# Where ScalarE and VectorE copy the turned attention weights in the first mixed step, and where TensorE turns them in the second

## What is computed

```python
scores = scale * q @ k.T;  scores = where(causal, -1e9, scores)
a = exp(scores - scores.max(-1));  a /= a.sum(-1) + 1e-9
local = a @ v
mem_out = (phi(q) @ M_prev) / (phi(q) . z_prev + 1e-6)
x = g * mem_out + (1 - g) * local            # rows of 512

h = x @ w_in                                  # layer 1, 512 -> 1024
sm = exp(h - h.max(-1));  sm /= sm.sum(-1) + 1e-9
solu = h * sm
ln = (solu - mean) / sqrt(var + 1e-6) * g_ln
x = ln @ w_out                                # 1024 -> 512

out = (sigmoid(x @ w_gate) * (x @ w_val)) @ w_out2   # layer 2
```

## Time and profile before

| What | Value |
|---|---|
| median of three runs | 836.41 us (835.51 to 836.73) |
| the profiled execution's own time | 835.18 us |
| its span | 833.4 us |
| time around the span | 1.8 us |
| TensorE (PE) busy | 814.7 us, 98% |
| VectorE (DVE) busy | 604.4 us, 73% |
| ScalarE (ACT) busy | 465.4 us, 56% |
| GpSimd (POOL) busy | 20.7 us, 2% |

### The profile page before, as it was taken

The page is one execution under the profiler, slowest core; times in us unless marked ns, Lnnn a source line. Parts: engine busy times, 40 slices in busy tenths (PEclk is TensorE's granted clock), DMA queues, the critical chain, the costliest instruction groups (busy, mean ns, idle before and its releaser), DMA issues.

```text
span 833.4 us, 15447 instructions
## 1 busy us (share of the span) xinstructions
PE 814.7 (98%) x5718; PEld 688.1 (83%) x5718; DVE 604.4 (73%) x1460; ACT 465.4 (56%) x965; POOL 20.7 (2%) x35
## 2 busy tenths in 40 slices
PE   7997999999999999999999999999999999999998
PEld 4555777777777778888899999999999999999997
DVE  7988888777777775686656777787677678666654
ACT  7988666666666653463535454564444465444443
POOL 1000000000000000111000000000000000000000
PEclk9999999999999999999999999999999999999999
DMA  7362011111111000100323011122111113111002
GB/s 217 93 194 61 17 52 53 53 52 54 53 50 39 26 17 15 52 1 1 101 77 126 26 51 52 52 61 98 45 52 50 52 42 111 51 52 51 26 1 77
DMA packets 67370, 48.99 MB, mean 59 GB/s; under 512 B 9568, under 2 KB 57952, under 8 KB 67296
## 3 DMA queue, kind: packets, MB, share of 16 engines
q1 hardware_dynamic: 67152, 47.74, 19.2%
q10 hardware_dynamic: 144, 0.26, 0.1%
HBM read 43.27 MB, written 4.72 MB: 58 GB/s over the span
## 4 chain that ended last, share of the span: by engine, by line
PE 89%; DVE 5%; SPq 2%; issue 2%; ACT 1%; DMA 1%; DVEq 0%; ACTq 0%
PE tt_bk L1622 10%; PE tt_bk L1624 10%; PE tt_bk L1623 10%; PE m_bk L1467 9%; PE s_bk L1491 7%; PE o_bk L1491 5%; PE tt_bk L1390 4%; PE s_bk L1674 3%; PE s_bk L1675 3%; PE s_bk L1673 3%; PE o_bk L1398 3%; PE s_bk L1326 3%; PE m_bk L1674 2%; PE m_bk L1675 2%; PE s_bk L1467 2%; PE m_bk L1673 2%
## 5 line engine op out<-in xcount | busy, mean ns | idle before, releaser
L1622 PE MATMUL tt_bk<-xc_hi,wc_hi 128*128 128x384 f32 x476 | 160.0, 336 | 0.0
L1624 PE MATMUL tt_bk<-xc_hi,wc_lo 128*128 128x384 f32 x476 | 160.0, 336 | 0.0
L1623 PE MATMUL tt_bk<-xc_lo,wc_hi 128*128 128x384 f32 x476 | 159.8, 336 | 0.0
L598 ACT ACTIVATE p_nat<-p_nat,negmax 128x512 f32<-128x512 f32 (+2 forms) x144 | 83.0, 578 | 46.6 <-DVE negmax L931 46.6
L1166 DVE TENSOR_TENSOR wc_lo<-wc_raw,wc_hi 128x768 fp32r<-128x768 f32 x72 | 78.3, 1088 | 31.9 <-ACT wc_hi L663 31.9
L1622 PEld LDWEIGHTS tt_bk<-xc_hi,wc_hi 128*128 128x128 f32 x476 | 89.4, 188 | 6.4 <-DVE c_u L1182 0.3
L1623 PEld LDWEIGHTS tt_bk<-xc_lo,wc_hi 128*128 128x128 f32 x476 | 89.4, 188 | 6.1
L1624 PEld LDWEIGHTS tt_bk<-xc_hi,wc_lo 128*128 128x128 f32 x476 | 89.4, 188 | 0.0
L663 ACT CAST wc_hi<-wc_raw 128x768 fp32r<-128x768 f32 x72 | 64.5, 946 | 1.3 <-DVE wc_raw L1160 1.3
L605 ACT COPY pT<-tt_bk 128x512 f32<-128x512 f32 (+1 forms) x87 | 46.0, 554 | 29.2 <-PE tt_bk L1390 27.8
L1390 PE MATMUL tt_bk<-ident,p_nat 128*128 128x128 f32 x400 | 56.0, 277 | 2.6 <-DVE pT L975 1.4
(11 more groups left out here) (219 smaller groups left out, 1773.7 us busy)
## 6 DMA issues: line engine op xcount, KB each, us to landing
wc_raw<-in_moe_w_val SPq DMA_DIRECT2D x36, 256.0 KB, 3.0
wc_raw<-in_moe_w_gate SPq DMA_DIRECT2D x36, 256.0 KB, 3.4
qkT<-in_q SPq DMA_DIRECT2D x15, 288.0 KB, 2.9
v_raw<-in_v SPq DMA_DIRECT2D x16, 256.0 KB, 2.7
qkT<-in_k SPq DMA_DIRECT2D x15, 256.0 KB, 3.2
out<-o_sb SPq DMA_DIRECT2D x15, 256.0 KB, 2.2
w_raw<-in_moe_w_out SPq DMA_DIRECT2D x12, 256.0 KB, 4.7
turned<-in_k SPq DMA_DIRECT2D x32, 72.0 KB, 2.6
```

The lines of the kernel that those rows point to most:

```text
L598: nc.scalar.activation(p_tile(g, tile), p_tile(g, tile), ACT.Exp, bias=negmax[:, n:n + 1], scale=-1.0, accum_out=den[:, n:n + 1]).then_inc ...
L1622: mm(o, hi[:, k, c, :], xc_hi[:, j, c, :], start=start and c == 0, stop=False, skip_group_check=True)
L1623: mm(o, hi[:, k, c, :], xc_lo[:, j, c, :], start=False, stop=False, skip_group_check=True)
L1624: last = mm(o, lo[:, k, c, :], xc_hi[:, j, c, :], start=False, stop=c == 1, skip_group_check=True)
```

## The change

In the first tile's step two copies of turned weights are placed ahead of the rows' maximum and its exponential. VectorE copies fill 3 before `split_w2` and `moe_max` (it did so behind them). Fill 4 is copied by ScalarE instead of VectorE, right behind its copy of fill 2 and ahead of `split_w2` of rows 5 and 6 and of `moe_exp`. TensorE's order in this step is the same as before.

In the second tile's step TensorE does all of `moe_hidden` first and then turns the fills among the groups of `moe_out`, where it had turned fills 0 and 1 and fills 2 and 3 among the hidden products. The orders of ScalarE and VectorE in this step stay as they were. The later steps are unchanged.

```diff
--- before.py
+++ after.py
@@ -71,7 +71,7 @@
     def act_fills(g):
         if g < HP:
             return list(range(NF))
-        return [0, 2, 5, 6] if g == HP else [0, 2, 4, 5, 6]
+        return [0, 2, 4, 5, 6]
 
     def dve_fills(g):
         return [n for n in range(NF) if n not in act_fills(g)]
@@ -807,12 +807,14 @@
                 if t == 0:
                     exp_tile(g, 8)
                 keep_pt(g - 1, 2)
+                if t == 0:
+                    keep_pt(g - 1, 4)
                 if t == 1:
                     feature_relu(g + 1)
                 for f in W2_HI_TILE.get(g, ()):
                     split_w2(f)
                 moe_exp(t)
-                if 4 in act_fills(g - 1):
+                if t:
                     keep_pt(g - 1, 4)
                 keep_pt(g - 1, 5)
                 if t == 0:
@@ -1095,12 +1097,13 @@
                     unit_max(g, 6)
                     split_w2(W2_LO_TILE[g][1])
                 keep_pt(g - 1, 1)
+                if t == 0:
+                    keep_pt(g - 1, 3)
                 if t < 2:
                     split_w2(W2_LO_TILE[g][2 if t == 0 else 0])
                 moe_max(t)
-                keep_pt(g - 1, 3)
-                if t == 0:
-                    keep_pt(g - 1, 4)
+                if t:
+                    keep_pt(g - 1, 3)
                 if t == 1:
                     split_w2(W2_LO_TILE[g][1])
                     split_w2(W2_LO_TILE[g][2])
@@ -1563,28 +1566,45 @@
                     scores(g, 2)
                 if t == 0:
                     scores(g, 3)
-                m = (15, 21) if t == 0 else (18, 24)
-                moe_hidden(t, 12, m[0])
-                turn_p(g - 1, 0)
-                turn_p(g - 1, 1)
-                moe_hidden(t, m[0], m[1])
-                turn_p(g - 1, 2)
-                turn_p(g - 1, 3)
+                if t != 1:
+                    m = (15, 21) if t == 0 else (18, 24)
+                    moe_hidden(t, 12, m[0])
+                    turn_p(g - 1, 0)
+                    turn_p(g - 1, 1)
+                    moe_hidden(t, m[0], m[1])
+                    turn_p(g - 1, 2)
+                    turn_p(g - 1, 3)
                 if t == 0:
                     moe_hidden(t, 21, 24)
-                if t:
+                if t > 1:
                     if g < PAIRS:
                         pe.wait_ge(max_ok, NU * g + NU - 1)
                     else:
                         pe.wait_ge(yt_ok, t - 1)
                     moe_out(t - 1, 0, 6)
-                turn_p(g - 1, 4)
-                turn_p(g - 1, 5)
-                if t:
+                if t != 1:
+                    turn_p(g - 1, 4)
+                    turn_p(g - 1, 5)
+                if t > 1:
                     moe_out(t - 1, 6, 12)
-                turn_p(g - 1, 6)
-                if t:
+                if t != 1:
+                    turn_p(g - 1, 6)
+                if t > 1:
                     moe_out(t - 1, 12, 24)
+                if t == 1:
+                    moe_hidden(t, 12, 24)
+                    turn_p(g - 1, 0)
+                    turn_p(g - 1, 1)
+                    pe.wait_ge(max_ok, NU * g + NU - 1)
+                    moe_out(0, 0, 6)
+                    turn_p(g - 1, 2)
+                    turn_p(g - 1, 3)
+                    moe_out(0, 6, 12)
+                    turn_p(g - 1, 4)
+                    turn_p(g - 1, 5)
+                    moe_out(0, 12, 18)
+                    turn_p(g - 1, 6)
+                    moe_out(0, 18, 24)
                 if t and g < PAIRS:
                     scores(g, 3)
```

## The result

| | Runs | Median | Lowest and highest |
|---|---|---|---|
| before | 22 | 836.14 us | 835.01 to 838.50 |
| after | 22 | 836.96 us | 835.74 to 840.54 |

The ratio of after to before is 1.0016, with an interval of 1.0009 to 1.0024. The time is 0.8 us longer by the medians. By the means it is 1.27 us longer (837.45 against 836.18), since six executions of the changed kernel lie between 838.38 and 840.54 us. They have a mean TensorE clock of 0.990 to 0.992. None of the 82 executions of the kernel before that were timed beside the experiments has that; the longest of these took 837.82 us. (One of the 22 above took 838.50 us, and its clock is not on record.) Without the six the mean is 836.71 us, 0.52 us above before. So there are two things to explain: a shift of about 0.6 us, and now and then 2 to 3 us more.

The account below looks back on a forecast made before the run. TensorE bounds the kernel, but ScalarE and VectorE bound the stretch from 80 to 97 us. Their 0.89 us delay less 0.30 us slack gives +0.59 us: 836.41 + 0.6 = 837.0 us, range 835.6 to 838.0.

Parts of the forecast that it names:

- ScalarE decides the side chain: First tile's step: ScalarE waits for fill 4, so `moe_exp` and the ScalarE/VectorE chain behind it come 0.89 us late.
- (a): Rival: side chain hardly delayed, as fill 4's copy is early or splits shorter; -0.3 us, down to -1.2; chance 0.13.
- (b): Rival: only `moe_max`'s delay of 0.43 us counts, the splits being hidden; +0.1 us, 836.5 us; chance 0.12.
- The chain passes on without loss: From `moe_rows` through `moe_square` and `x_lo` to `y_nat`, no slack eats the 0.89 us delay.
- `weighted` waits for the copies of fills 5 and 6, and comes 0.45 us late: TensorE starts `weighted` at about 81.9 instead of 81.45 us, held by ScalarE's copies behind `moe_exp`.
- A new wait ahead of `moe_out`, 0.5 us: Second tile's step: `moe_out` waits for unit 5's maximum, at 95.66 us, while fills 0 and 1 are turned by 95.2.
- The slack at `y_nat`, 0.30 us: Ahead of TensorE's turn of `y_nat`, 0.30 us of slack takes up part of the side chain's delay.
- The sum of +0.59: Whole kernel: side chain's delay of 0.89 us less 0.30 us of slack at `y_nat`; nothing of the removed waits survives.
- The clock stays at 1.00: Around the longer wait ahead of `weighted`, TensorE's granted clock stays full, as between 77 and 82 us; cost nothing.
- rival (d): Rival: the clock falls after TensorE's longer idle time before `weighted`, costing 1.5 us; +2.1 us, 838.5 us; chance 0.03.

Follow-up runs that it names:

- e3: The changed kernel plus seven matmuls with unread results in TensorE's wait ahead of `weighted`; 837.00 us, ratio 1.0005.
- e4: The changed kernel, but ScalarE copies fill 4 behind the two splits of `w_out` and ahead of `moe_exp`; 836.23 us, ratio 1.0001.
- e2: The kernel before with only TensorE's new order in the second tile's step; 836.00 us, ratio 0.9996.
- a1: The changed kernel, unaltered, traced once more; one run, 839.96 us.
- e7: The kernel before with only the first tile's change, plus seven unread matmuls in TensorE's wait ahead of `weighted`; 836.86 us, ratio 1.0007.
- e8: As e5, and ScalarE also copies `y_nat` ahead of the exponential of `q` in the second tile's step; 835.86 us, ratio 0.9995.
- e1: The kernel before with only the first tile's change of ScalarE and VectorE, TensorE's order as before; 837.06 us, ratio 1.0012.
- e5: On e2, ScalarE makes `x_hi` of the second tile ahead of the last split of `w_out`; 835.94 us, ratio 0.9992.
- e6: On e4, VectorE's copy of fill 3 also goes back behind `moe_max`; fill 4 stays with ScalarE; 836.48 us, ratio 1.0001.
- a2: The changed kernel, unaltered, traced another time; one run, 838.44 us.
- e9: The changed kernel with a third split of `w_out` (row 7) ahead of `moe_exp`, lengthening the wait ahead of `weighted`; 838.49 us, ratio 1.0026.

## Why the prediction was right, and where it was not

The time was 836.96 us where 837.0 was forecast, within 0.2% of before and inside the range. That the two agree to 0.04 us is luck: the forecast started from 836.41 us, the median of three runs, and the median of 22 is 836.14, so the measured difference of the medians is 0.82 us and not 0.6. What bears the forecast out is the shift of 0.61 us in e3, where the clock doesn't fall. The steps fared as follows.

**ScalarE decides the side chain.** Right. The idle stretch ahead of the copy was 0.96 us (forecast 1.0 to 1.1), `moe_exp` was 0.89 us late (forecast 0.89), `moe_max` 0.43 (forecast 0.43), and they do not add up: e4 removes ScalarE's part and leaves VectorE's. Rivals (a) and (b) needed a delay of ScalarE that isn't there, and fall.

**The chain passes on without loss.** Right. The copy of `y_nat` begins 27.98 us behind fill 4 in e3, and began 27.09 behind it (104.40 - 77.31): the whole 0.89 us.

**`weighted` waits for the copies of fills 5 and 6, and comes 0.45 us late.** This step failed. It comes 0.87 us late (5.01 against 81.45 - 77.31 = 4.14), and its releaser is `moe_rows`, not a copy. In the second tile's step TensorE has a wait for `u_ok` ahead of `weighted` (in `step`, for `t` = 1, behind those for the copies), and I read only the waits for the copies. Before, `moe_rows` ended at 81.23 (80.01 + 1.22) and `weighted` started at 81.45, behind it as well. So this start hangs on the side chain, and moves with it: 0.87 of the 0.89 us. The open wait is 2.11 us, not 1.7. For the sum this made no difference, since the wait at `y_nat` swallows either.

**A new wait ahead of `moe_out`, 0.5 us.** Half right: in e3, where the clock doesn't fall, `moe_out` starts at 95.99 us, 18.41 behind fill 4, and the forecast was 95.71 - 77.31 = 18.40. But TensorE came to it later than forecast, with the turning of fills 0 and 1 begun at 95.03, and so the wait is 0.3 us (its 0.69 us before the next instruction taken off). In the profiled execution of after it has no wait there at all, since the low clock had made it later still. The reordering is worth 0.28 us by itself (e2), where the forecast had 0.9 up to this point and 0.30 behind `y_nat`.

**The slack at `y_nat`, 0.30 us.** It was 0.37 (e2): the prediction took 0.12 us from the end of the copy to the turn, and in e2 and e3 it is 0.05 to 0.06 (27.65 to 27.71 and 28.55 to 28.60 behind fill 4). The turn of `y_nat` is thus 0.52 us late in e3. Another 0.09 us is lost before the third tile's hidden products, 0.06 of it in the turn of `memo` (0.49 us to the next group, before 0.43) and 0.03 in the group `tt_bk<-mz,phi` (0.72, before 0.69); why these take longer is not shown. The sum of +0.59 is measured as +0.61, and that it comes so close is luck in part: the slack was taken 0.07 us too small, and the 0.09 us were not in the sum.

**The clock stays at 1.00.** This term was mis-sized. I gave a fall 0.03, on the row of 77 to 82 us, and with an open wait of 1.7 to 1.9 us. The wait was longer, and the fall came in all three traces of the changed kernel. It cost 0.9 to 2.6 us where rival (d) had 1.5, and is the whole of what after has over e3. By the mean clock of the executions it is in six of the 22, and by its trace in the profiled one (0.995) too, so in at least seven. The median stays at the forecast in spite of it, and the mean, 837.45 us, is 0.45 us above it.

The rows of before could not exclude the fall. In the stretch of the same length ahead of `weighted` TensorE was busy for 2.05 of 3.40 us, with the clock at 1.00 behind it:

```profile
78.00:81.40 3.40, 2.05 (x15) 0.94 (x15) 3.15 (x7) 2.38 (x5) 0.00 (x0) 1.00 0.00 0
81.40:86.00 4.60, 4.60 (x69) 3.29 (x65) 3.16 (x11) 4.21 (x9) 0.55 (x1) 1.00 0.02 5
```

The change takes the wait for fill 3 out of the middle of that idle time and adds it at the end, with the delay on top, so that 1.31 of 3.40 us are left. And the stretch at a clock of 0.54 from 12.7 to 16.0 us that the prediction quotes stood right behind a single wait of 2.62 us, which neither the rows nor the prediction show:

```profile
12.75 1.98 PE L1326 MATMUL s_bk<-qkT 64*64 64x384 f32 x16 [2.62 <-DVE negmax L931]
```

So before had one wait of 1.44 us without a fall and one of 2.62 us with one, and the expected wait of 1.7 to 1.9 us lay between the two. The row from 77 to 82 us spoke for the first alone, and a chance of 0.03 was too small for that. (All traces here have such a wait in the start-up, of 1.97 to 3.07 us, and a clock of 0.50 to 0.61 from 12.7 to 16.0.) The Trainium skill names this mechanism ("TensorE: Matmul & The Clock Gate", Part 1: The HAM clock gate), and the traces agree with it in direction: in a1 1.33 of 3.40 us of work up to the end of the wait, then 0.50 for some 6 us, and full rate again only behind work.

**What stays open.** Whether an execution of after at a mean clock of 0.993 to 0.996 has the fall. Executions of before lie there too, and the traces show why the mean can't tell. From 10 to 20 us the clock is either 0.83 or 0.55 to 0.61. Without a fall at the wait the first goes with a mean of 0.997 or 0.998 (before, e2, e3, e4, e7, e8), the second with 0.994 (e1, e5, e6). With a fall the first gives 0.995 (after), the second 0.989 to 0.992 (a1, a2, e9). So by these traces the mark of 0.992 catches only executions that have both, and seven of 22 is a lower bound. The traced fall and the low mean clock go together in a1 (0.990) and a2 (0.992), the only executions at that level that have a trace. Why one execution falls at the same 2.11 us wait and another (e1's trace) doesn't is not shown either. Nor is it shown whether the length of the one wait or all the idle time around it decides: from before to after both grow, and no run changes one alone.

## What to carry to other kernels

When a copy is moved ahead of other work on its engine, ask when its input is ready: if that is later than the engine gets there, all that is queued behind pays the idle time and the copy, less what it would have waited anyway: here 0.96 + 0.48 - 0.57 us, about 0.9 us for a copy of 0.5. Before you say what an instruction waits for, list every wait ahead of it in the code, and check by the trace which of them comes last. And where a change makes one wait of TensorE longer, compare it with the waits of the trace you have and with the granted clock behind each, and take more than one trace of the changed kernel: such a wait can cost the clock as well. Independent matmuls put into it kept the clock here.

## What the runs showed of the hardware

- TensorE's granted clock went from 1.00 to 0.50, that is from 2.4 to 1.2 GHz, at the end of a single wait of 2.11 us (a1 and a2; in the profile of after the mean of the 4.6 us behind the wait is 0.63). This was in the middle of the kernel and in three of the four traces that have this wait; TensorE was busy for 1.29 to 1.33 of the 3.40 us up to its end in all four, and the fourth (e1, 1.32) stays at 1.00.
- In the start-up the same is seen in all 13 traces: a wait of 1.97 us (e1) to 3.07 us (e4) that ends at 12.1 to 13.1 us, and a granted clock of 0.50 to 0.61 from 12.7 to 16.0 us.
- It stays low while TensorE is busy without a gap: in a1 2.00 of 2.00 us busy from 86 to 88 and from 88 to 90, at 0.50 in both. The group of 24 matmuls takes 4.53 us there, against 2.38 at 1.00.
- With seven extra matmuls in the wait (2.90 of 3.20 us busy in e3) the clock stays at 1.00 in both traces (e3, e7), and none of the 22 executions has a mean clock as low as 0.992; 9 of the 33 with the wait open do.
